# Linear attention and two MoE layers on one core: attention's items in a new order, the opening's lists and banks, and a second home for K transposed

## What is computed

```python
q_s = exp(q - max(q, -1)); q_s = q_s / (sum(q_s, -1) + 1e-9)      # over the 64 of a head
k_s = exp(k - max(k, 2));  k_s = k_s / (sum(k_s, 2) + 1e-9)       # over the 576 of the sequence
kv = einsum('bhsd,bhse->bhde', k_s, v)
x = einsum('bhsd,bhde->bhse', q_s, kv)                            # 8 batches, 8 heads, 576, 64
x = x.transpose(0, 2, 1, 3).reshape(4608, 512)
g = x @ w_gate; x = (g * sigmoid(g) * (x @ w_val)) @ w_out        # 512 -> 1536 -> 512
h = maximum(maximum(x @ w1, x @ w2), x @ w3); out = h @ w_out2    # 512 -> 768 -> 512
```

## Time and profile before

| | us |
|---|---|
| three runs | 1554.91, 1556.95, 1561.85; median 1556.95 |
| profiled execution | 1555.91 |
| its span, first to last instruction | 1554.1 |
| PE busy in it | 1492.3 (96%) |
| DVE, ACT, POOL busy | 823.5, 544.9, 655.5 |
| mean granted TensorE clock | 0.987 of full |

### The profile page before, as it was taken

One profiled execution on the slowest core, in us unless ns is written; L12 is line 12 of the kernel. 1 busy time (PEld: TensorE's weight loads), 2 busy tenths in 40 slices (PEclk: granted clock), 3 DMA queues, 4 the chain that ended last, 5 costly groups with the idle time before them and its releaser, 6 DMA issues.

```text
span 1554.1 us, 20750 instructions
## 1 busy us (share of the span) xinstructions
PE 1492.3 (96%) x7002; PEld 1237.2 (80%) x7002; DVE 823.5 (53%) x1344; ACT 544.9 (35%) x996; POOL 655.5 (42%) x523
## 2 busy tenths in 40 slices
PE   8687998989999999999999999999999999999999
PEld 7475877878778788888888888888788888888898
DVE  7535575674766654755455444633543543443444
ACT  5434353443443423333233222443422322322222
POOL 5546575565732324432143132687813223222211
PEclk9989999999999999999999999999999999999999
DMA  8978766667586665665556564297676576575585
GB/s 241 316 239 259 241 226 223 214 221 271 179 260 212 206 210 184 215 185 180 189 184 198 175 210 150 75 336 266 234 249 195 167 246 196 170 228 185 176 306 196
DMA packets 180903, 334.56 MB, mean 215 GB/s; under 512 B 13376, under 2 KB 68672, under 8 KB 173120
## 3 DMA queue, kind: packets, MB, share of 16 engines
q1 hardware_dynamic: 175616, 323.80, 63.7%
q10 hardware_dynamic: 5184, 9.44, 2.0%
HBM read 256.90 MB, written 76.28 MB: 214 GB/s over the span
## 4 chain that ended last, share of the span: by engine, by line
PE 84%; POOL 5%; DVE 4%; issue 2%; ACT 2%; DMA 2%; SPq 0%; ACTq 0%; DVEq 0%; POOLq 0%
PE round L1575 12%; PE round L1577 12%; PE round L1578 12%; PE y_bank L1603 8%; PE y_bank L1604 8%; PE y_bank L1605 8%; PE third_bank L1575 5%; PE third_bank L1578 5%; PE third_bank L1577 5%; PE att_bank L1508 2%; PE round L1468 1%; PE round L1469 1%; PE round L1470 1%; PE att_bank L1513 1%; POOL h L601 1%
## 5 line engine op out<-in xcount | busy, mean ns | idle before, releaser
L601 POOL TENSOR_TENSOR h<-hid,h 128x512 fp32r<-128x512 f32 (+1 forms) x156 | 202.1, 1297 | 490.1 <-ACT h L1081 489.8
L1575 PE MATMUL round<-xops,wring 128*128 128x512 f32 (+1 forms) x930 | 358.5, 386 | 3.4 <-POOL wring L585 2.1
L1577 PE MATMUL round<-xops,wring 128*128 128x512 f32 (+1 forms) x930 | 354.0, 381 | 0.0
L1578 PE MATMUL round<-xops,wring 128*128 128x512 f32 (+1 forms) x930 | 353.9, 381 | 0.0
L1371 DVE TENSOR_TENSOR y_sb<-y_sb,y_bank 128x512 f32<-128x512 f32 x232 | 158.5, 685 | 235.1 <-PE y_bank L1605 234.2
L1575 PEld LDWEIGHTS round<-xops,wring 128*128 128x128 f32 x930 | 175.7, 189 | 40.0 <-issue 4.0
L1578 PEld LDWEIGHTS round<-xops,wring 128*128 128x128 f32 x930 | 175.5, 189 | 33.7
L1577 PEld LDWEIGHTS round<-xops,wring 128*128 128x128 f32 x930 | 175.7, 189 | 31.1
L1081 ACT ACTIVATE h<-hid 128x512 fp32r<-128x512 f32 (+1 forms) x156 | 95.4, 612 | 199.3 <-DVE hid L1332 117.5
L1603 PE MATMUL y_bank<-h,wout 128*128 128x512 f32 x384 | 152.3, 397 | 0.0
L1604 PE MATMUL y_bank<-h,wout 128*128 128x512 f32 x384 | 150.0, 391 | 0.0
(11 more groups left out here) (161 smaller groups left out, 2597.2 us busy)
## 6 DMA issues: line engine op xcount, KB each, us to landing
wring<-kept SPq DMA_DIRECT2D x216, 512.0 KB, 4.1
wout<-kept_o SPq DMA_DIRECT2D x36, 1024.0 KB, 6.2
wring<-kept SPq DMA_DIRECT2D x108, 256.0 KB, 3.1
stage<-x_dram SPq DMA_DIRECT2D x32, 512.0 KB, 6.3
kept<-wring SPq DMA_DIRECT2D x9, 1792.0 KB, 9.5
kept<-wring SPq DMA_DIRECT2D x12, 1024.0 KB, 5.7
raw<-w_g SPq DMA_DIRECT2D x21, 512.0 KB, 5.1
x_dram<-stage SPq DMA_DIRECT2D x16, 576.0 KB, 3.6
```

The costliest lines, as they stand in the source:

```text
L601: pool.tensor_tensor(h[:, t, 1, 0:cols], hid[:, t, 0:cols], h[:, t, 0, 0:cols].bitcast(F32), ALU.subtract).then_inc(h_lo_ready, 1)
L1575: pe.matmul(dst[:, 0:g.cols], hi, x1, start=(i in (1, 5) and c == 0), stop=False, skip_group_check=True)
L1577: pe.matmul(dst[:, 0:g.cols], hi, x2, start=False, stop=False, skip_group_check=True)
L1578: mm = pe.matmul(dst[:, 0:g.cols], lo, x1, start=False, stop=(c == 1), skip_group_check=True)
```

## The change

1. Batches 1 to 7 get another order of items (`LATER_ITEMS`: QT 0 before KV 0, QT 1 before KV 1, QT 2 before KV 2) and new places for items and maxima.
2. The opening's three lists are reordered: weights 0 to 2 come later on ACT and POOL, `max_q` 3 to 5 and `sum_q` 3 to 5 later on DVE; the first two weight loads are issued after KM 2.
3. In the opening the items use five banks in turn.
4. X of the first block is split straight from its bank; in batch 0 only the last 64 columns are copied to `x_out` and stored.
5. K transposed of batches 1 and 2 has two buffers in turn (`kt_sb` and a part of `y_sb`).

```diff
-ITEMS = [
+FIRST_ITEMS = [
...
+LATER_ITEMS = [
+    ("KM", 0), ("KM", 1), ("QT", 0), ("KV", 0), ("KM", 2), ("QT", 1), ("KV", 1), ("KM", 3), ("QT", 2),
+    ("KV", 2), ("KV", 3), ("X", 0), ("X", 1), ("X", 2), ("X", 3), ("QT", 3), ("QT", 4), ("QT", 5),
+    ("X", 4), ("X", 5), ("X", 6), ("X", 7),
+]
...
-GAPS = [4, 7, 8, 9, 10, 11, 13, 14, 15, 16, 17, 18.5, 19.3, 20.1, 20.9, 22, 23, 24, 26.6, 27.5, 28.4, 29.3]
-MAX_K = [2.5, 5.5, 8.5, 11.5]
-MAX_Q = [2.6, 8.6, 11.6, 14.6, 17, 19.2]
+GAPS = [3.2, 6.2, 6.6, 7.4, 9.2, 9.7, 10.4, 12.2, 12.7, 13.4, 16, 18, 18.8, 19.6, 20.4, 21.4, 22.4, 23.6,
+        26.2, 27.1, 28, 28.9]
+MAX_K = [1.5, 4.5, 7.5, 10.5]
+MAX_Q = [0.8, 3.4, 6.4, 10.9, 13.8, 16.8]
...
 SCALAR_0 = [
-    ("exp_q", 0), ("KM", 0), ("exp_q", 1), ("weight", 0), ("KM", 1), ("QT", 0), ("KV", 0),
-    ("exp_q", 2), ("weight", 1), ("KM", 2), ("exp_q", 3), ("KV", 1), ("weight", 2), ("KM", 3),
-    ("QT", 1), ("KV", 2), ("exp_q", 4), ("QT", 2), ("exp_q", 5), ("KV", 3), ("split_x", 0),
...
+    ("exp_q", 0), ("KM", 0), ("exp_q", 1), ("KM", 1), ("KV", 0), ("QT", 0), ("exp_q", 2), ("KM", 2),
+    ("KV", 1), ("KM", 3), ("weight", 0), ("exp_q", 3), ("QT", 1), ("KV", 2), ("QT", 2), ("weight", 1),
+    ("exp_q", 4), ("KV", 3), ("weight", 2), ("exp_q", 5), ("split_x", 0), ("split_x", 1), ("split_x", 2),
...
 VECTOR_0 = [
     ("max_q", 0), ("max_k", 0), ("max_q", 1), ("KM", 0), ("sum_q", 0), ("max_k", 1), ("max_q", 2),
-    ("KM", 1), ("max_k", 2), ("KV", 0), ("sum_q", 1), ("QT", 0), ("max_q", 3), ("KM", 2), ("max_k", 3),
-    ("KV", 1), ("sum_q", 2), ("KM", 3), ("max_q", 4), ("sum_q", 3), ("KV", 2), ("max_q", 5), ("QT", 1),
...
+    ("KM", 1), ("max_k", 2), ("KV", 0), ("sum_q", 1), ("KM", 2), ("QT", 0), ("max_k", 3), ("sum_q", 2),
+    ("KV", 1), ("KM", 3), ("max_q", 3), ("KV", 2), ("QT", 1), ("sum_q", 3), ("max_q", 4), ("QT", 2),
+    ("KV", 3), ("max_q", 5), ("sum_q", 4), ("split_x", 0), ("split_x", 1), ("split_x", 2), ("split_x", 3),
...
+        def kt_place(b, p):
+            if b == 0:
+                return (0, 1, 2, 0)[p]
+            return p % 2 if b < 3 else 0
...
+        att_first = att_banks + [rounds[2]] + y_banks
...
+            return att_first[n % 5] if b == 0 else att_banks[n % 2]
...
             def store_x(b, half):
...
+                skip = BLOCK - HALF if b == 0 else 0
                 first = (2 * b + half) * HALF
-                sp.dma_start(x_dram[:, :, first:first + HALF], x_out[half][:, :, :]).then_inc(x_stored[half], 16)
+                sp.dma_start(x_dram[:, :, first + skip:first + HALF], x_out[half][:, :, skip:])\
...
             load_kt(1, 0)
+            load_kt(1, 1)
...
-            store_x(0, 0)
...
             def split_x_first(m):
                 p, first, cols = first_block_cols(m)
-                act.wait_ge(item_out_dve, items_before(item_no("X", m) + 1))
-                act.activation(x_hi[:, p, first:first + cols], x_out[m // PAIRS][:, p, 0:cols], ACT.Copy).then_inc(x_hi_ready, 1)
+                n = item_no(0, "X", m)
+                act.wait_ge(item_done, n + 1)
+                act.activation(x_hi[:, p, first:first + cols], att_bank(0, n)[:, 0:cols], ACT.Copy)\
...
-                if (step, n) == ("KM", 0):
+                if (step, n) == ("KM", 2):
                     load_unit(0)
                     load_unit(1)
...
-                if not (b == 0 and n < 2):
-                    before = n - 2 if n >= 2 else n - 2 + NITEMS
+                if b or n >= 5:
+                    before = n - 5 if b == 0 else n - 2 if n >= 2 else n - 2 + NITEMS
```

More of the change, by code:

```diff
@@ L274, in whole_order, with item_no, dve_items @@
     return order
[L277 to L282, removed]
+def item_no(b, kind, n):
+    return ITEMS[b].index((kind, n))
+def dve_items(b, n):
+    count = 0
+    for of in range(b + 1):
+        for kind, m in ITEMS[of][:n] if of == b else ITEMS[of]:
+            count += kind == "QT" or (kind == "X" and (of > 0 or m >= PAIRS))
+    return count
 FILLS = PAIRS + 1
-DVE_ITEMS = items_before(NITEMS)
 def split_no(n, c):
@@ L367, in v_tile @@
             return v_sb[:, p % 2, :, :]
+        def kt_place(b, p):
+            if b == 0:
+                return (0, 1, 2, 0)[p]
+            return p % 2 if b < 3 else 0
         def kt_tile(b, p):
-            if b == 0 and p in (1, 2):
-                return y_sb[:, 2 * p - 2:2 * p, :].rearrange("p a b -> p (a b)")[:, 0:SEQ]
+            place = kt_place(b, p)
+            if place:
+                return y_sb[:, 2 * place - 2:2 * place, :].rearrange("p a b -> p (a b)")[:, 0:SEQ]
             return kt_sb[:, :]
@@ L447, in program @@
         y_stored = [sem(f"y_stored{n}") for n in range(8)]
[L449 removed]
+        kt_in = [sem(f"kt_in{n}") for n in range(3)]
         k_in = [sem(f"k_in{n}") for n in range(2)]
@@ L656, in third_after @@
             def third_after(e):
-                if e[0] == "item" and ITEMS[e[2]][0] == "KV":
-                    split_kv(e[1], ITEMS[e[2]][1])
+                if e[0] == "item" and ITEMS[e[1]][e[2]][0] == "KV":
+                    split_kv(e[1], ITEMS[e[1]][e[2]][1])
             for step, n in POOL_0:
@@ L726, in after_max_k @@
             def after_max_k(b, p):
-                if p < PAIRS - 1 and b:
-                    load_kt(b, p + 1)
-                elif p == PAIRS - 1 and b + 1 < BATCH:
-                    load_kt(b + 1, 0)
+                for n in range(PAIRS * b + p + 1, PAIRS * BATCH):
+                    if kt_place(*divmod(n, PAIRS)) == kt_place(b, p):
+                        load_kt(*divmod(n, PAIRS))
+                        return
             def load_raw(n):
@@ L1160, in next_after @@
                     first_tanh(e[1])
-                elif e[0] == "item" and ITEMS[e[2]][0] == "QT":
+                elif e[0] == "item" and ITEMS[e[1]][e[2]][0] == "QT":
                     item_out(e[1], e[2])
@@ L1176, in second_after @@
                     first_split_h(e[1])
-                elif e[0] == "item" and ITEMS[e[2]][0] in ("KM", "KV"):
+                elif e[0] == "item" and ITEMS[e[1]][e[2]][0] in ("KM", "KV"):
                     item_out(e[1], e[2])
@@ L1248, in item_out @@
                     half, p = divmod(m, PAIRS)
-                    if p == 0 and b:
-                        dve.wait_ge(x_stored[half], 16 * b)
+                    skip = BLOCK - HALF if b == 0 else 0
+                    if p == 0 and b + half > 1:
+                        dve.wait_ge(x_stored[half], 16 * (b - 1 + half))
                     if p == 0 and half == 0 and b >= 3:
@@ L1403, in next_after @@
                     first_value(e[1])
-                elif e[0] == "item" and ITEMS[e[2]][0] != "QT":
+                elif e[0] == "item" and ITEMS[e[1]][e[2]][0] != "QT":
                     item_out(e[1], e[2])
@@ L1415, in second_after @@
             def second_after(e):
-                if e[0] == "item" and ITEMS[e[2]][0] == "QT":
+                if e[0] == "item" and ITEMS[e[1]][e[2]][0] == "QT":
                     item_out(e[1], e[2])
@@ L1496, in item @@
                         pe.wait_ge(item_out_act, PAIRS * of + number + 1)
+                    elif of == 0 and last == "X" and number < PAIRS:
+                        pe.wait_ge(x_lo_first, number + 1)
                     else:
-                        pe.wait_ge(item_out_dve, DVE_ITEMS * of + items_before(before + 1))
+                        pe.wait_ge(item_out_dve, dve_items(of, before + 1))
                 if kind == "KM":
```

80 lines of the change are left out of this document (44 added, 36 removed), and 3 rows, old and new, of the table VECTOR_0.

## The result

The changed kernel takes **1540.68 us** (median, 1540.10 to 1541.31), the kernel before 1555.93 (1553.94 to 1561.85) beside it: a ratio of **0.9896, 95% interval 0.9868 to 0.9924**, 15.3 us faster. The forecast was 1523.0, so less than half of the 33.9 us came. The time is inside the range of 1508 to 1542, near its slow end, where the rival "loads and banks give half back" stood (1536).

What follows compares the result with a forecast made beforehand. Ahead of 600 us, TensorE's idle time and low clock were taken as the loss. Savings 2.3 + 1.6 + 5.6 + 7.0 + 1.0 + 16.4 = 33.9 us from 1555.9 gave 1522.0, 1523 on the median's scale; range 1508 to 1542.

Steps and rivals of the forecast that it cites:

- loads and banks give half back: Rival: transfers limit batches 1 and 2 (5 gained, not 12.6), late bank waits run longer (11, not 16.4); 1536, chance 0.20.
- What bounds the kernel: TensorE is always busy from 600 us on; ahead of that, idle time and the low clock lose time that can be saved.
- Batches 3 to 6, -16.4: Six waits for POOL's scaled Q vanish (-14.9), low clock behind four (-6.5), new KM-to-KV bank waits cost 5.0; range -10 to -21.
- The opening, -2.3: Up to gate 0: later weights, fewer X copies and more banks bring gate 0 2.3 us earlier; range 0 to -6.
- walked through queue by queue, X3's split ends some 2.1 us earlier: In the opening: following each engine's queue with weights moved later, X3's split ends some 2.1 us earlier.
- tanh of gate 0, -1.6: At gate 0: tanh stands directly behind U6 on ACT, no longer behind U7 and U8; 1.6 us saved, range 0 to -3.
- Batch 1, -5.6: Batch 1's stretch: idle time falls to 12.7 (-2.2), low-clock loss to 2.7 (-3.4); second k_t buffer removes k_max waits; 0 to -12.
- Batch 2, -7.0: Batch 2's stretch: idle time plus low-clock loss falls from 14.8 to 7.8 us; range -2 to -11.
- The same walk gives 1.4, 0.4, 2.9 (KV 2 behind K of pair 3) and 1.5, and one stretch at the low clock, 1.6: Batch 2: four TensorE waits left, starting with KV0's, plus one low-clock loss, found by following the queues; 7.8 us in all.
- To pair 0, -1.0: Up to pair 0: X7 of batch 2 ahead of val 9 gives two units more for x's store, load, sums; 0 to -2.
- What would show it: Signs in the later profile: late scale waits under 1 us, KV waits 0.5 to 2.5, batch 1's first KM near 41.5.
- It is wrong if the low clock follows the KV waits: Sign against the forecast: TensorE at its lower clock behind KV items' waits for DVE's subtraction.

Runs made afterwards that it cites:

- the second trace of the changed kernel: The changed kernel run once more without any edit, as measure for other kernels, against the kernel before: 0.9899, 1542.73 us.

## Why the prediction was partly right

*What bounds the kernel.* Right. From 770 us on the lead stays at 15.8 to 16.0 (between 650 and 760 it dips, to 13.6 at the least, and comes back), and nothing behind batch 7 moved.

*Batches 3 to 6, -16.4.* Right in mechanism and nearly in size. The list of TensorE's waits over 205 to 560 us has none for POOL's scale, and the new KM to KV waits are there in four places, each batch's KV 1:

```profile
PE att_bank L1545 <- DVE k_sb L1264: 5.2, 4, 2.5
PE round L1612 <- DVE c L1338: 2.8, 1, 2.8
```

5.2 us against a forecast of 5.0. None of the four stretches at the low clock of before is left; two new ones, at 211 behind the wait for c and at 228 behind the wait of 2.54, belong to the start of pair 0. Behind the 4th sum the lead grew by 14.1.

*The opening, -2.3.* It took two edits for one. With the old lists, the five banks and the direct split alone end the splits of X at 37.8, 1.8 us ahead of before (39.6); the new lists give that back (39.8). The step that failed here is "walked through queue by queue, X3's split ends some 2.1 us earlier": it ended at 32.5, before at 32.4, and with the old lists at 30.7. The walk followed the moved weights and not the subtraction for Q 5, which was moved too. One term was better than said. The direct split's form was put at no cost; it takes 0.46 us for 288 columns, where the form of before, with both operands in SBUF, took 0.44 to 1.08, while DVE reached it behind a copy of 0.45:

```profile
29.24 1.08 DVE L1203 TENSOR_TENSOR xops<-stage,xops 128x288 fp32r<-128x288 f32 x1
```

*tanh of gate 0, -1.6.* Right, and too small: from the end of X's splits to gate 0 it was 4.2 us before and is 1.3 now, -2.9. With the old order in batches 1 to 7 it is 4.6 again (split to 40.2, gate 0 at 44.84), with it in batch 1 alone 4.2: ACT splits U7 and U8, each behind its load, ahead of tanh 0.

*Batch 1, -5.6.* The sum was right (5.8), the shares were not, so that it fits is in part luck. The forecast's waits came partly: KM 1 3.3 for 4.6, KV 1 and KV 2 0.8 and 1.8 for 1.7 and 3.0, and KV 0 1.5, which had no term. K of pair 3 was no wait here. The low clock cost 4.6 us of work, at 50 to 58 and 71 to 75 us, for the 2.7 forecast (6.1 before). The second buffer is worth 3 with the new order. With the old order and the second buffer the lead rises by 8.0 between gate 0 and gate 5 (-0.3 to 7.7), more than the 5.8 of the new order; what the new order gives, 1 to 3 us at the end, lies ahead of gate 0, where it is 3.0 us earlier.

*Batch 2, -7.0.* **The step that failed.** "The same walk gives 1.4, 0.4, 2.9 (KV 2 behind K of pair 3) and 1.5, and one stretch at the low clock, 1.6". The wait was named, but its size came from three loads of the late batches, which landed 2.6 to 4.9 us after their issue. Here K's second part landed 7.9 us after its issue, 8.3 after that of the first (124.58 to 132.9). The wait of KV 2 was 4.28 for 2.9, the low clock behind it took 2.6 us of work in place of 1.6, and DVE's 5.82 us pushed what followed. The trace of before had the nearer rows: in the loop over the gates K's parts landed up to 6.9 us after their issue, in batch 2 6.3 and 6.5 for those issued at 135.84 and 136.52. Why K lands so late in some places stays open. It isn't the size of the store ahead of it, as its halving showed, and not the share of the DMA engines alone: it was 0.93 from 124 to 133 us here, and 1.05 from 430 to 435 us before, where K, issued at 431.52, landed within 5.3 us. The walk also left out pair 0's first split of x, which the old order met at another place, and so X 2's 4.75. Moving KM 3 to KV 3 behind the landing took both waits away and gave 7 us of lead, 5 by the ratios.

*To pair 0, -1.0.* Wrong in sign. "X7 now lies ahead of val 9, two units more" holds, but X 7 came at about 172 us, not at 160, and the new places put batch 3's first steps into DVE's queue where pair 0 begins: +2.7. The wait of 2.83 wasn't among the terms; the earlier trace rows showed the small one of before, and I didn't ask what the new places put ahead of it.

*The rivals.* The outcome lies nearest to the first, 1536, though not by its mechanism: transfers didn't bound batch 1 (lowering the share from 0.98 to 0.90 in 42 to 110 us gave 1.1 us, within the noise) and the late bank waits came as forecast. Of its sentence "loads give half back" one load remains. The Trainium skill's warning of small runs, "DMA: Bandwidth & Descriptors" (Specifications), was weighed at no cost, and nothing here speaks against that: no wait in the trace is for the store of X.

*What would show it.* Held: no scale wait over 1 us in batches 3 to 6, KV waits of 0.7 to 2.5 there, tanh 0 behind U6, no wait for k_t in batches 1 and 2 (7.8 us before; the 1.8 that are left lie in the opening). Not held: first KM item of batch 1 at 42.64 (41.5), X 7 of batch 2 near 160 (172). "It is wrong if the low clock follows the KV waits" was the sign to look for, and it came at 132 us.

## What to carry to other kernels

Take the price of a load from rows of the stretch where it will be issued, and take the longest; the parts of one load of K landed up to 4.9 us after their issue in the rows that the forecast used, up to 6.9 in the loop of the kernel before, and 7.9 in the changed one. When places of many steps move together, walk each engine's queue at the seams too, where the new order meets work that the change doesn't touch: X 2's wait in batch 2 and the wait at pair 0's first sum lay there. And a gain that an undone edit doesn't return can still be had: putting batch 2's old order back gave 1 to 2 us, moving a few items in the new one gave 5. A single trace moves by 1.7 us with each stretch at the low clock, which may come or not behind the same wait; look at the clock before a cause is sought in the change.

## What the runs showed of the hardware

DVE and POOL hold each other up, by more than I had allowed for. The low half of h takes 0.69 us alone and took 3.81 while POOL ran these without a gap:

```profile
148.93 1.04 POOL L581 TENSOR_TENSOR q_sb<-q_sb,q_rec 96x512 f32<-96x512 f32 x1
149.93 1.26 POOL L564 TENSOR_TENSOR xops<-hid,xops 128x512 fp32r<-128x512 f32 x1
151.15 1.26 POOL L564 TENSOR_TENSOR wout<-hid,wout 128x512 fp32r<-128x512 f32 x1
```

It began 0.2 us into the first of them (149.15) and ended at 152.96, 0.6 us after the end of the third; in the second trace of the changed kernel it took 3.80. The other way round POOL is the slower: here DVE's low half of h began first and took its 0.68 us, and POOL's scaling, 1.04 us above, took 1.48:

```profile
112.23 0.68 DVE L1306 TENSOR_TENSOR h<-hid,h 128x512 fp32r<-128x512 f32 x1
...
112.33 1.48 POOL L581 TENSOR_TENSOR q_sb<-q_sb,q_rec 96x512 f32<-96x512 f32 x1
```

The Trainium skill, "SBUF — State Buffer" (Who interferes with whom), says that a DVE instruction with two SBUF inputs contends with a GpSimd instruction that reads SBUF, and calls the shared port pair an exclusive lock. Both rows agree, and the first shows that DVE can be held up by three instructions in a row, not by one. By the same section a DVE instruction with at most one SBUF input, outside of its two-port modes, is free of it; the direct splits, at 0.38 to 0.46 us with POOL busy beside them, agree. So the form that saves a copy also ends this contention for the split.
